# Feed-forward by pairs of channel tiles over a whole batch, with h from seven block products in place of eight in two of three input tiles

## The reference

```
state[t] = alpha[t] * state[t-1] + k[t] (x) v[t];  y[t] = q[t] . state[t]      # 4 batches, 8 heads, 768 tokens, 48 wide
x = y, heads side by side                                                     # [4, 768, 384]
theta = x @ w_theta; u = x + w_tok_r @ (x cos theta) + w_tok_i @ (x sin theta); x = u + relu(u @ w_ch)
h = relu(x @ w_in)                                                            # [4, 768, 1024]
conv = c0*h[t-1] + c1*h[t] + c2*h[t+1]                                        # per channel
out = (h * sigmoid(conv)) @ w_out                                             # [4, 768, 384]
```

## Time and profile before

| | us |
|---|---|
| median of three executions | 523.84 |
| the profiled execution | 523.99 |
| its span, first to last instruction | 522.3 |
| TensorE busy | 514.5 (99% of the span) |
| VectorE busy | 441.5 (85%) |
| ScalarE busy | 277.8 (53%) |
| GpSimd busy | 72.0 (14%) |

### The profile page before, as it was taken

One profiled execution on the slowest core, in us unless ns is written; L12 is line 12 of the kernel. 1 busy time (PEld: TensorE's weight loads), 2 busy tenths in 40 slices (PEclk: granted clock), 3 DMA queues, 4 the chain that ended last, 5 costly groups with the idle time before them and its releaser, 6 DMA issues.

```text
span 522.3 us, 11326 instructions
## 1 busy us (share of the span) xinstructions
PE 514.5 (99%) x4070; PEld 505.9 (97%) x4070; DVE 441.5 (85%) x801; ACT 277.8 (53%) x583; POOL 72.0 (14%) x65
## 2 busy tenths in 40 slices
PE   7999999999999999999999999999999999999997
PEld 7999898999999999999999999999999999999997
DVE  8999997999898659775888786998898898989884
ACT  3989887755533433433336552664545454545453
POOL 5988984000000000000000000000000000000000
PEclk9999999999999999999999999999999999999999
DMA  8999997999050405127020012101112020201011
GB/s 323 330 319 338 348 310 198 273 309 262 11 215 1 90 2 178 45 64 234 3 92 0 1 46 92 47 31 62 48 42 75 15 90 0 90 0 47 1 46 45
DMA packets 39613, 61.68 MB, mean 118 GB/s; under 512 B 6160, under 2 KB 28688, under 8 KB 39568
## 3 DMA queue, kind: packets, MB, share of 16 engines
q1 hardware_dynamic: 36448, 56.36, 33.9%
q10 hardware_dynamic: 3120, 4.72, 2.5%
HBM read 46.92 MB, written 14.16 MB: 117 GB/s over the span
## 4 chain that ended last, share of the span: by engine, by line
PE 95%; DMA 1%; SPq 1%; issue 1%; ACT 1%; DVE 1%; ACTq 0%; POOL 0%; POOLq 0%
PE y_bank L1531 29%; PE y_bank L1589 19%; PE theta_bank L1576 10%; PE x_bank L1576 10%; PE y_bank L1561 7%; PE x_bank L1518 7%; PE weighed L1438 4%; PE x_sum L1396 4%; PE x_sum L1411 2%; PE turned L1423 2%; DMA q_in<-in_q_rows 1%; PE turned L1443 1%; SPq L790 1%; PE x_sum L1382 0%; SPq L785 0%
## 5 line engine op out<-in xcount | busy, mean ns | idle before, releaser
L1589 PE MATMUL y_bank<-first_w,z 128*128 128x384 f32 x576 | 109.6, 335 | 0.0
L1589 PEld LDWEIGHTS y_bank<-first_w,z 128*128 128x128 f32 x576 | 101.2, 188 | 0.0
L1531 PE MATMUL y_bank<-first_w,z 128*128 128x384 f32 x432 | 76.9, 335 | 0.3 <-issue 0.3
L1531 PE MATMUL y_bank<-rest_w,z 128*128 128x384 f32 x432 | 76.2, 334 | 0.0
L1531 PEld LDWEIGHTS y_bank<-first_w,z 128*128 128x128 f32 x432 | 75.0, 188 | 0.5 <-issue 0.5
L1531 PEld LDWEIGHTS y_bank<-rest_w,z 128*128 128x128 f32 x432 | 75.0, 188 | 0.1
L1341 DVE TENSOR_SCALAR x_rows<-out_rows,taps 128x384 f32<-128x384 f32 x64 | 26.8, 419 | 19.5 <-ACT out_rows L1103 19.4
L1103 ACT ACTIVATE out_rows<-theta_bank 128x386 f32<-128x386 f32 x32 | 15.8, 494 | 50.9 <-PE theta_bank L1576 50.9
L1518 PE MATMUL x_bank<-theta_w,x_t 128*128 128x384 f32 x216 | 41.5, 336 | 0.3 <-DVE x_t L1224 0.3
L1344 DVE SCALAR_TENSOR_TENSOR x_rows<-out_rows,taps,x_rows 128x384 f32<-128x384 f32 x64 | 39.6, 619 | 2.3
L1348 DVE SCALAR_TENSOR_TENSOR z_full<-out_rows,taps,x_rows 128x384 f32<-128x384 f32 x64 | 39.6, 619 | 2.3
(11 more groups left out here) (126 smaller groups left out, 927.5 us busy)
## 6 DMA issues: line engine op xcount, KB each, us to landing
a_in<-in_a_rows SPq DMA_DIRECT2D x15, 390.0 KB, 6.1
k_in<-in_k_rows SPq DMA_DIRECT2D x15, 384.0 KB, 5.9
q_in<-in_q_rows SPq DMA_DIRECT2D x14, 384.0 KB, 5.7
v_in<-in_v_tokens SPq DMA_DIRECT2D x16, 288.0 KB, 4.7
y<-x_even SPq DMA_DIRECT2D x7, 576.0 KB, 3.3
x_blocks<-x_scratch SPq DMA_DIRECT2D x12, 288.0 KB, 5.7
u_scratch<-u_sum ACTq DMA_DIRECT2D x6, 576.0 KB, 3.3
u_first<-u_scratch SPq DMA_DIRECT2D x4, 577.5 KB, 4.3
```

Source lines behind the costliest of these rows:

```text
L1531: ins = pe.matmul(y_bank[2 * d + half][:, 0:HALF], z[s % 2][part][zp][:, d * P:(d + 1) * P], mixing_w(part, wp, s)[:, half_tokens(half)], ...
L1589: ins = pe.matmul(out_bank[half][t][:, 0:MODEL], g[k % 4][gp][:, t * P:(t + 1) * P], out_w[wp][f], start=f == 0 and i == 0, stop=f == FF_T ...
```

## The change

The feed-forward's unit becomes a pair of channel tiles (an even and an odd one) over a whole batch of 768 tokens. There are 16 such steps. A step's four blocks of h (even or odd tile, first or second 384 tokens) come from eight stages on TensorE, `STAGES`. With A for blocks of w_in and B for blocks of u (two of the three input tiles each), seven products of sums and differences of blocks stand for the eight block products (Strassen's scheme in Winograd's form); the third input tile is added as before (`c0`, `c1`).

```diff
-LAG = 4
+STAGES = ((("a11", "b11"),), (("s2", "t2"),), (("a12", "b21"), ("even", "c0")), (("s3", "t3"),), (("s1", "t1"),),
+          (("a22", "t4"), ("odd", "c0")), (("s4", "b22"), ("even", "c1")), (("odd", "c1"),))
+BETWEEN = (2, 1, 1, 2, 2, 2, 1, 1)
 TensorE:
-        def front(b, k):
-            h_done.before(pe, n, 2)
-            for i, (wp, up) in enumerate(PASSES):
-                for d in range(MODEL_TILES):
-                    ins = pe.matmul(h_bank[k % 2][:, 0:WIDE], in_w[wp][:, d, f * P:(f + 1) * P], u_c[half][up][d], ...
+        def stage(n, i):
+            if q == 0 and i == 0:
+                u_split.done(pe, b)
+            if i == 0:
+                gathered.done(pe, n - 1, 5)
+            if i == 1:
+                gathered.done(pe, n - 1, 6)
+            if i == 2:
+                p1_kept.done(pe, n)
+            if i == 3:
+                gathered.done(pe, n, 1)
+            if i == 4:
+                even_first.done(pe, n)
+            if i == 5:
+                gathered.done(pe, n, 2)
+            if i == 6:
+                gathered.done(pe, n, 3)
+            if i == 7:
+                gathered.done(pe, n, 4)
+            terms = [(ff_w[w][wp][:, q, :], ff_u[u][b % 2][up]) for w, u in STAGES[i] for wp, up in PASSES]
+            for m, (w, u) in enumerate(terms):
+                ins = pe.matmul(h_bank[i % 2][:, 0:HALF], w, u, start=m == 0 and i not in (2, 6), stop=m == len(terms) - 1, ...)
+        def step(k):
+            for i, between in enumerate(BETWEEN if k + 3 < FF_STEPS else ...):
+                stage(k + 2, i)
+                for _ in range(between):
+                    back_group(k, *next(groups))
 GpSimd:
+        def combine_u(b):
+            first, second, third, fourth = (u_raw[b][:, d, half_tokens(half)] for d in range(2) for half in range(2))
+            u_split.done(pool, b, 2)
+            pool.tensor_tensor(first, second, first, ALU.subtract).then_inc(u_combined.sem, 1)
+            ...
+        def prepare_u(k):
+            b, phase = prepared_in(k)
+            if phase == 0:
+                split_u(b, 0)
+            if phase == 1:
+                combine_u(b)
+            if phase == 2:
+                split_u(b, 1)
+                split_u(b, 2)
+        def split_g(n, j):
+            g_high[j].done(pool, n)
+            added_up.done(pool, n - 2)
+            pool.tensor_tensor(g[n % 2][j][1], conv[j], g[n % 2][j][0].bitcast(F32), ALU.subtract).then_inc(g_low[j].sem, 1)
+        def step(k):
+            prepare_u(k)
+            if k + 1 < FF_STEPS - 1:
+                split_g(k + 1, 0)
+                split_g(k + 1, 1)
 ScalarE:
+        def round_u(b, m):
+            if m == 2:
+                u_combined.done(act, b)
+            act.activation(high, raw, ACT.Copy).then_inc(u_rounded.sem, 1)
+        def step(k):
+            n, m = k + 2, k + 1
+            relu_odd(m)
+            keep_p1(n)
+            if q == 0 and b > 0:
+                for t in range(HALF_TILES, T):
+                    evacuate(b - 1, t)
+            conv1(m, 1)
+            prepare_u(k, False)
+            relu_even_first(n)
+            gate(m, 0)
+            gate(m, 1)
+            if q == FF_PAIRS - 1 and 0 <= b < LAST:
+                for t in range(HALF_TILES):
+                    evacuate(b, t)
+            prepare_u(k, True)
+            round_g(m, 0)
+            round_g(m, 1)
+            relu_even_second(n)
+            conv1(n, 0)
 VectorE:
+        def step(k):
+            conv2(m, 0)
+            gather_u2(n)
+            conv3(m, 0)
+            conv2(m, 1)
+            gather_u3(n)
+            conv3(m, 1)
+            gather_c22(n)
+            apply_gate(m, 0)
+            gather_odd_first(n)
+            apply_gate(m, 1)
+            gather_even_second(n)
+            gather_odd_second(n)
```

More of the change, by code:

```diff
@@ L352, in mix_batch @@
                 do.mix(b, s)
+            if s == T - 1 and not last:
                 do.sums(b)
@@ L384, in mix_batch @@
             do.send(b, 1)
[L386 to L403, removed]
     for i in range(PAIRS):
@@ L408, in program @@
     for b in range(BATCH):
[L409 to L424, removed]
+        mix_batch(b, b == BATCH - 1)
+    for n in range(2):
+        do.begin(n)
+    for k in range(FF_STEPS):
+        do.step(k)
 def layer(nc, ctx, a_rows, k_rows, q_rows, v_rows, v_tokens, w_theta, w_tok_r, w_tok_i, w_ch, w_in, taps_in, w_out,
@@ L1566, in join @@
-        def join():
-            first.done(pe, LAST_TILE)
-        def front(b, k):
-            n, f, half = b * K + k, k % FF_TILES, k // FF_TILES
-            if f == 0:
-                c_low.done(pe, 2 * b + half)
-            h_done.before(pe, n, 2)
-            for i, (wp, up) in enumerate(PASSES):
-                for d in range(MODEL_TILES):
-                    ins = pe.matmul(h_bank[k % 2][:, 0:WIDE], in_w[wp][:, d, f * P:(f + 1) * P], u_c[half][up][d],
-                                    start=i == 0 and d == 0, stop=i == 2 and d == MODEL_TILES - 1)
-            ins.then_inc(h_made.sem, 1)
@@ L1593, in _, with end_group @@
-        for t in (theta_made, mixed, multiplied, h_made, added_up):
+        def end_group(b, half, m):
+            d, i = divmod(m, len(PASSES))
+            wp, up = PASSES[i]
+            if m == 0:
+                u_low.done(pe, b, 3 * half + 3)
+                if b == 0:
+                    piece_low.done(pe, len(pieces) - 1)
+            for c in range(MODEL_TILES):
+                ins = pe.matmul(y_bank[2 * d + half][:, 0:HALF], channel_w[wp][:, c, d * P:(d + 1) * P],
+                                u_part[up][:, c, half_tokens(half)],
+                                start=i == 0 and c == 0, stop=i == 2 and c == MODEL_TILES - 1)
+            if i == 2:
+                ins.then_inc(multiplied.sem, 1)
@@ new lines, in _ @@
+        END_GROUPS = MODEL_TILES * len(PASSES)
+        def end(b, half):
+            for m in range(END_GROUPS):
+                end_group(b, half, m)
+        def stage(n, i):
+            b, q = divmod(n, FF_PAIRS)
+            if n == 0 and i == 0:
+                first.done(pe, LAST_TILE)
+                pe.wait_ge(w_low, N_W)
+            if q == 0 and i == 0:
[4 more added lines that the diff above has]
+                gathered.done(pe, n - 1, 6)
+            if i == 2:
+                p1_kept.done(pe, n)
[11 more added lines that the diff above has]
+            for m, (w, u) in enumerate(terms):
+                ins = pe.matmul(h_bank[i % 2][:, 0:HALF], w, u, start=m == 0 and i not in (2, 6), stop=m == len(terms) - 1,
+                                skip_group_check=True)
+            ins.then_inc(h_made.sem, 1)
```

649 lines of the change are left out of this document (428 added, 221 removed).

## The result

The changed kernel takes **553.5 us** (median of four executions, 552.81 to 554.21), the kernel before 523.91 us beside it: ratio 1.0563, 95% interval 1.0543 to 1.0584. The direction was as predicted, the size was not: 18.5 us above the forecast of 535, and 12.5 above the end of the range.

A forecast was written before the change was run, and what follows sets the result against it. TensorE, busy 99% of the span, was taken as the bound. 523.99 us less 9.0 saved gave 515.0; plus 20.7 for order and contention gave 535.7, so about 535 us, range 516 to 541.

The forecast's parts named there:

- TensorE's saving: Feed-forward: 69 matmuls a step, 12.04 us against 12.60; sixteen steps save 9.0 us, giving 515.0 us if nothing waits.
- The signs in the profile: Feed-forward after the change: TensorE idle in batches' first steps behind relu, longer VectorE taps and gates, plain steps 12.1 to 12.3 us.
- phase 0: Last step of a batch: low part of g late into the next step, 0.2 us by order, 1.0 us with contention.
- phase 2: Feed-forward step with 5.1 us of u's preparation on GpSimd: no loss by order, 2.0 to 2.5 us with contention.
- The order, 7.0 us: Feed-forward batch starts: waits from work order without contention, 1.9 us for each of two transitions plus 3.2 us for the first.
- The contention: Feed-forward: VectorE operations with two SBUF inputs stand still until GpSimd's operation ends; 20.7 to 25.4 us in all.
- the lower: First step of a batch: GpSimd's sums run on in one piece, stage 4 is 2.4 to 2.6 us late; 20.7 us in all.
- The discarded layout: First step of a batch: GpSimd waits for VectorE too, sums end at 10.1, stage 4 is 4.6 us late; 25.4 us in all.
- The mixing, "I price it at nothing": Mixing: some 34 us of added GpSimd work costs nothing as VectorE idled 1 to 2 us a token tile; 3 us kept for upper end.
- Order alone: Rival for the feed-forward: contention hardly shows, only work order makes TensorE wait; 522.0 us, range 519 to 525, chance 0.22.
- All hidden: Rival for the feed-forward: no engine over 80% full, nothing waits; 515.0 us, range 514 to 519, chance 0.19.
- The pace: Rival on TensorE: bank start and stop flags or shorter matmul runs cost its 0.175 us pace; about 524 us, chance 0.02.

The follow-up runs named there:

- the bound of 519.1 us: Changed kernel with GpSimd's arithmetic in mixing and feed-forward replaced by writes, and ScalarE rounding the sums of u later: 519.1 us, ratio 0.9903.
- With writes: Changed kernel with GpSimd's arithmetic in feed-forward and mixing replaced by memsets of the same places, same waits and order: 526.6 us, ratio 1.0072.
- the best is at 536.2 us: Changed kernel with mixing work spread, u's preparation on VectorE and its sums rounded later; low part of g stays on GpSimd: 536.2 us, ratio 1.0240.
- the two runs with writes: Changed kernel with GpSimd's arithmetic replaced by writes, in the feed-forward only: 532.6 us; in the mixing too: 526.6 us.

## Why the prediction was right and wrong

**TensorE's saving: right.** 69 matmuls take 11.96 us (predicted 12.04). The sum of 515.0 without a wait is borne out: the bound of 519.1 us has 1.8 + 1.1 + 1.1 us over 11.96 left in steps 0, 4 and 8, 4.0 us in all, so 515.1. (Its feed-forward started at 307.4 and not at 308.0, so 515.7 from the same start.)

**The signs in the profile: right but for one.** Relu of the even first half as releaser, the rounding that waits for L1026 ahead of it, phase 0 late by 1.0 us (six waits for z, 0.4 and 1.0 to 1.7), taps and gates longer than alone, and a plain step of 12.2 us (11 and 12; 12.1 to 12.3 predicted), though the plain steps behind phase 2 took 12.9. One of the signs of being wrong came as well: TensorE waits at the join, 2.7 us, where less than 1 us more than before was expected.

**The order, 7.0 us: at most a little too low.** With writes the three steps are 3.9, 3.4 and 3.4 us over 11.96, so 10.7 us. Part of this is the substitute. Its chain in step 0, three low parts and four sums, takes 10.2 us; from the arithmetic's own lengths (1.84 and 0.93 to 1.02 us) I estimate 9.2 to 9.6. That is 2 to 3 us over three steps, which leaves an estimated 8 to 9. The prediction had 1.69 us for each low part, where the fp32r output takes 1.84.

**The contention: the step that failed.** The prediction laid out the transition twice and took the lower, "since in the rows GpSimd is the one that never waits". In the changed kernel it waits: the sums took 1.74, 1.41, 1.59 and 1.59 us on average, not 0.93, and in step 4 the last of them ended, at 404.72, 10.2 us after the step's first matmul. The discarded layout said 10.1.

```profile
394.52 0.68 PE L1877 MATMUL x_bank<-theta_w,in_w 128*128 128x384 f32 x3
...
403.13 1.59 POOL L1026 TENSOR_TENSOR out_rows<-out_rows 128x384 f32<-128x384 f32 x1
```

The wait for relu was then 4.25 and 4.21 us in steps 4 and 8, where that layout had 4.6 and the chosen one 2.4 to 2.6. (In step 0 it was 2.46 us, but there TensorE had already lost 1.74 us for the low part of g and 0.90 for u_sum.) The rows of before could not show that GpSimd waits: in them GpSimd's operation had always begun first. With the upper layout the sum is 515.0 + 25.4 = 540.4 us. The Trainium skill (SBUF — State Buffer, "Who interferes with whom") states it symmetrically: whichever instruction is issued first holds the shared ports to its end, and the other is blocked; a GpSimd instruction that only writes doesn't contend with a VectorE instruction that has two SBUF inputs. The runs agree with both: 1.63 of 1.76 us blocked is the standstill but for 0.13, and beside writes the groups stood at 1.01 and 0.95 us.

**The mixing, "I price it at nothing": failed.** 5.9 us. The reason given, VectorE's idle 1 to 2 us a token tile, holds for work spread over tiles; here three operations fell between two angles, in one place, and cost 2.7 us of waiting and 1.7 of clock; the sums of w_in cost 1.2 elsewhere. The prediction had also weighed only operations with two inputs. L1441 and L1451 have one input, in SBUF, and went from 0.36 to 1.53 and 1.89 us. The Trainium skill (SBUF — State Buffer, "Who interferes with whom") has the rule: TENSOR_SCALAR can run in a fast form that takes both ports, and then contends with GpSimd. The trace agrees, by these lengths.

**The clock: missing from the sum.** Four times after a long wait TensorE ran at the lower level. One is counted in the mixing's 5.9 us; three lie in the feed-forward, 3 x 1.7 = 5.1 us.

Upper layout, mixing and clock: 540.4 + 5.9 + 5.1 = 551.4 us, against 553.4 for the profiled execution. By the lengths of the steps, against 11.96 us (10.7 for steps -2 and -1), most of the 2.0 us left can be placed. Phases 0 to 2 with the step after them lost 24.3 us besides the clock, where 24.2 was laid out; all the others lost 2.7 (the last stretch against its 28.7 us in the run of 519.1), where 1.2 was. That the split fits so well is in part luck, since the steps after phase 2 (12.9 us) were laid out as plain ones, and which wait makes them longer was not shown.

**The rivals.** Order alone (522.0): the order as it is gives 526.6 without contention, an estimated 2 to 3 us of it the substitute's, so without contention the change would have been worth about nothing, not 1.8 us. All hidden (515.0): not reached by any run. The pace: no loss. None of the versions with all of the arithmetic beats the kernel before; the best is at 536.2 us. Whether one exists was not settled.

## What to carry to other kernels

Before work is moved to an idle engine, look at what it reads and at whose instructions run at the same time: an idle GpSimd is no free room while VectorE works on two SBUF inputs, and what counts is the share of time in which both have such work. Where two layouts differ only in who waits, and no row shows it, take the dearer one for the sum. And look at each rounding or copy that stands ahead of the reader of a bank: here its place in one list was worth some 11 us, more than the 9 us that the saved matmuls were worth.

## What was not expected of the hardware

A wait can cost more than its length. In the mixing and the feed-forward of all runs, kernel before included, the granted clock fell to 1.2 GHz after 20 of 23 idle stretches of TensorE of 2.5 to 4.3 us, and after 6 of 19 of 1.7 to 2.2 us. Each fall cost 1.7 us. So the same wait can end either way: step 0 of the two runs with writes has the same waits (1.8 us for relu), and the clock after them was 0.66 and 0.50 in one and 1.00 in the other, which is 1.6 us of step length. Even 2.7 us for z in the mixing, and once 3.4 us, passed without a fall. Two versions of a kernel that differ by less than 2 us may differ in this alone.

The second case is the turn-taking. Two engines with several such operations in a row don't overlap but alternate, and nothing in the profile is called a wait: each operation appears with its own length plus what the other's had still to run when it began, less 0.1 to 0.2 us. In step 0 above, GpSimd's L1026 began 0.74 us before the end of VectorE's L1568 and took 1.59 us for 0.93; VectorE's L1568 began 0.46 us before the end of GpSimd's L1024 and took 1.28 for 1.01.
